# Local attention scores: the order of the small matmuls, and the half of PSUM each head's scores go to

## What is computed

```python
# branch 1: q, k and v averaged over 4 positions, full softmax attention on 144 positions, result repeated 4 times
out_up = np.repeat(sm_attn(q_d, k_d, v_d), 4, axis=2)
# branch 2: full resolution, but only |i - j| < 4
scores = np.where(mask, scale * np.matmul(q, k.transpose(0, 1, 3, 2)), -1e9)
out_local = np.matmul(softmax(scores), v)
x = (out_up + out_local) as (2304 tokens, 512 channels)
y = (silu(x @ w_gate) * (x @ w_val)) @ w_out            # hidden width 1536
out = relu(y @ w2_in) ** 2 @ w2_out                      # hidden width 2048
```

## Time and profile before

| | |
|---|---|
| median of 3 executions | 917.95 us (914.18 to 918.93) |
| the profiled execution's own time | 917.95 us |
| its span, first to last instruction | 916.2 us |
| TensorE (PE) busy | 897.9 us, 98% |
| VectorE / ScalarE / GpSimd busy | 650.9 / 400.5 / 219.4 us |

### The profile page before, as it was taken

The page is one execution under the profiler, slowest core; times in us unless marked ns, Lnnn a source line. Parts: engine busy times, 40 slices in busy tenths (PEclk is TensorE's granted clock), DMA queues, the critical chain, the costliest instruction groups (busy, mean ns, idle before and its releaser), DMA issues.

```text
span 916.2 us, 17274 instructions
## 1 busy us (share of the span) xinstructions
PE 897.9 (98%) x6762; PEld 868.0 (95%) x6762; DVE 650.9 (71%) x1112; ACT 400.5 (44%) x733; POOL 219.4 (24%) x278
## 2 busy tenths in 40 slices
PE   7899999999999999999999999999999999999998
PEld 4589899999999999999999999999999999999998
DVE  7786665653677575887575899585879585878774
ACT  3565454553446252555343545151535241525331
POOL 5884465533352001502000313000403000202000
PEclk9999999999999999999999999999999999999999
DMA  9954333222132020321312220010332020221422
GB/s 233 243 155 118 109 96 108 68 78 95 47 104 70 1 70 24 104 81 35 104 35 92 82 104 1 1 35 2 104 103 70 1 70 1 81 81 40 133 70 70
DMA packets 70881, 71.38 MB, mean 78 GB/s; under 512 B 27280, under 2 KB 58000, under 8 KB 70800
## 3 DMA queue, kind: packets, MB, share of 16 engines
q1 hardware_dynamic: 68496, 65.55, 24.1%
q10 hardware_dynamic: 2304, 4.72, 1.4%
HBM read 56.10 MB, written 14.16 MB: 77 GB/s over the span
## 4 chain that ended last, share of the span: by engine, by line
PE 83%; DVE 6%; ACT 3%; SPq 2%; issue 2%; POOL 2%; DMA 1%; DVEq 0%; ACTq 0%; POOLq 0%
PE mlp_ps L978 13%; PE mlp_ps L980 12%; PE mlp_ps L979 12%; PE sc L978 5%; PE sc L980 5%; PE sc L979 5%; PE xp L978 4%; PE xp L980 4%; PE xp L979 4%; PE sd L978 3%; PE sd L980 3%; PE sd L979 2%; PE tr L978 2%; PE tr L980 2%; PE tr L979 2%
## 5 line engine op out<-in xcount | busy, mean ns | idle before, releaser
L1391 ACT ACTIVATE wh_hi<-hbuf 128x384 fp32r<-128x384 f32 x144 | 70.8, 522 | 79.4 <-DVE hbuf L1677 57.1
L694 POOL TENSOR_TENSOR w_raw<-w_raw 128x256 f32<-128x256 f32 x16 | 13.9, 867 | 355.7 <-DMA w_raw<-w_in 355.7
L1685 DVE TENSOR_TENSOR wh_lo<-hbuf,wh_hi 128x384 fp32r<-128x384 f32 x144 | 76.6, 561 | 24.5 <-ACT wh_hi L1391 21.1
L1640 DVE TENSOR_TENSOR ring<-ring_raw,ring 128x768 fp32r<-128x768 f32 x96 | 91.3, 975 | 0.0
L1340 ACT ACTIVATE ring<-ring_raw 128x768 fp32r<-128x768 f32 x96 | 75.3, 836 | 28.9 <-DVE ring_raw L1634 28.5
L978 PE MATMUL mlp_ps<-ring,w_hi 128*128 128x384 f32 x240 | 80.3, 334 | 0.4 <-ACT snap L1371 0.4
L980 PE MATMUL mlp_ps<-ring,w_lo 128*128 128x384 f32 x240 | 80.2, 334 | 0.0
L979 PE MATMUL mlp_ps<-ring,w_hi 128*128 128x384 f32 x240 | 80.2, 334 | 0.0
L978 PE MATMUL mlp_ps<-wh_hi,w_hi 128*128 128x384 f32 x216 | 73.0, 338 | 2.2 <-DVE ypart L1745 1.2
L979 PE MATMUL mlp_ps<-wh_lo,w_hi 128*128 128x384 f32 x216 | 72.2, 334 | 0.0
L980 PE MATMUL sc<-wh_hi,w_lo 128*128 128x384 f32 x216 | 72.2, 334 | 0.0
(11 more groups left out here) (208 smaller groups left out, 2648.3 us busy)
## 6 DMA issues: line engine op xcount, KB each, us to landing
ring_raw<-x_whole SPq DMA_DIRECT2D x24, 384.0 KB, 3.6
ring_raw<-y_whole SPq DMA_DIRECT2D x24, 384.0 KB, 3.6
qk_sb<-qT SPq DMA_DIRECT2D x16, 288.0 KB, 3.3
qk_sb<-kT SPq DMA_DIRECT2D x16, 288.0 KB, 3.9
v_grp<-v SPq DMA_DIRECT2D x32, 144.0 KB
x_whole<-x_f ACTq DMA_DIRECT2D x16, 288.0 KB, 2.4
y_whole<-ypart SPq DMA_DIRECT2D x3, 1536.0 KB, 6.3
v_win<-v SPq DMA_DIRECT2D x64, 64.0 KB, 2.9
```

The lines of the kernel that those rows point to most:

```text
L694: nc.gpsimd.tensor_tensor(block(5), block(7), block(4), ALU.add).then_inc(s_usum[i], 1)
L1391: nc.scalar.activation(hi[:, f, t, :], hbuf[:, e, :], ACT.Copy).then_inc(s_shhi, 1)
L1640: nc.vector.tensor_tensor(ring[:, SLOTS[g][p], 1, :, :], whole(g, p), ring[:, SLOTS[g][p], 0, :, :].bitcast(F32), ALU.subtract).then_inc(s ...
L1685: nc.vector.tensor_tensor(lo[:, f, t, :], hbuf[:, e, :], hi[:, f, t, :].bitcast(F32), ALU.subtract)\
```

## The change

`local_place` goes away. The scores of head h are now always on partitions 64h onwards, in both banks. The loop over the 20 score matmuls becomes: first all j with head 0 taking t = 0 and head 1 taking t = 1, then all j with head 0 taking t = 1 and head 1 taking t = 0. The values' matmuls keep their order and read their probabilities from the columns that belong to the new place.

```diff
-        def local_place(h, t):
-
-            return h ^ t
-
...
-            for j in range(TJ):
-                for t in range(2):
+            for swap in range(2):
+                for j in range(TJ):
                     for h in range(2):
-                        rows, place = slice(64 * h, 64 * h + 64), 64 * local_place(h, t)
+                        t = h ^ swap
+                        rows = slice(64 * h, 64 * h + 64)
                         s, w = query_at(t, j), window_at(t, j)
-                        last = nc.tensor.matmul(sc[place:place + QT, loc_tile(t, j)],
+                        last = nc.tensor.matmul(sc[64 * h:64 * h + QT, loc_tile(t, j)],
                                                 qk_sb[rows, ring, 0, s:s + QT], qk_sb[rows, ring, 1, w:w + KWIN],
                                                 start=False, stop=(j == TJ - 1))
...
-                        rows, first = slice(64 * t, 64 * t + 64), P * j + 64 * local_place(h, t)
+                        rows = slice(64 * t, 64 * t + 64)
                         last = nc.tensor.matmul(local_bank(i, t)[64 * h:64 * h + 64, QT * j:QT * (j + 1)],
                                                 v_win[rows, ring, j, h, :],
-                                                probsT_l[rows, ring, first:first + QT],
+                                                probsT_l[rows, ring, P * j + 64 * h:P * j + 64 * h + QT],
                                                 start=True, stop=True)
```

## The result

The changed kernel takes 920.96 us in the median (919.59 to 922.07, 11 executions), the kernel before 915.86 us (914.15 to 920.18, 11 executions). The ratio is 1.0053, with a 95% interval from 1.0041 to 1.0065: 4.9 us slower (3.8 to 6.0). The forecast was 924.2 us from 917.95 us, 6.3 us slower. The sign and the mechanism were right, the size was about 1.4 us too large. The measured 920.96 us lies only 0.5 us above the lower end of the forecast range, because the base was taken 2 us too high; the growth itself lies well inside.

What follows compares the result with a forecast made beforehand. TensorE, busy 98% of the span, was taken as the bound after 44 us: 917.95 us plus 6.3 for eleven pairs in the slots, with the opening and the rest at 0, gave 924.2 us; range 920.5 to 929 us.

Steps and rivals of the forecast that it cites:

- Four at once, then two: Local scores: a pair's 40 records go from 10 groups of four to 20 of two, adding 0.57 us a pair.
- The slots: Eleven pairs after 43.9 us, between matmuls that wait for nothing: 11 x 0.57 = 6.3 us added.
- there the addition counts in full: In the slots after 43.9 us, all added score time was to lengthen the kernel: 6.3 us.
- added, but swallowed: Rival, after 44 us: TensorE's waits shrink by 4.6 us, leaving 1.7 us added, 919.7 us; chance 0.08.
- The opening: Pairs 0 to 4, before the slots: 3.4 us of new work hidden by waits, costed at 0.
- The matmul at 43.91 us: At the first slot, waiting for GpSimd's chain without TensorE's part: was to stay there within 0.3 us.
- Two at a time already: Rival, local scores: heads sharing a bank already take turns, so the change costs 0, 918.0 us; chance 0.07.
- Weights no longer ahead: Rival, score groups: weight loads not ahead of the stream, 0.10 us a group, 15.4 us, 933.4 us; chance 0.04.
- The time of before: Whole kernel before the change: 917.95 us, taken as the base of the forecast.

Runs made afterwards that it cites:

- e2: Kernel before with only the changed places (head h always on partitions 64h), loop order as before: ratio 1.0059, 1.12 us for a pair.
- e3: Kernel before with only the changed loop order, places as before: ratio 1.0035, 0.961 us for a pair.
- e4: Kernel before with, inside each j, four quarters still used but neighbours always in different banks: ratio 1.0009, 0.576 us for a pair.
- e7: Kernel before with loop order changed so that ten records in a row go to one quarter of the array: ratio 1.0147.
- e6: Kernel before with the changed places and order for pairs 0 to 4 alone, those of the opening: ratio 0.9997.
- e1: The changed kernel again, unaltered, for a second profile: ratio 1.0041 to the kernel before, median 920.58 us.
- e10: The kernel of e5 once more, against the kernel before: ratio 1.0054.
- e5: Kernel before with the changed places and order for pairs 5 to 15 alone, those of the slots: ratio 1.0068.
- e8: The kernel before again, unaltered, for a second profile: 0.575 us for a pair, 149.74 us from pair 5 to pair 15.
- e11: Kernel before with 8 filler matmuls behind the last values of round 4, ahead of the wait at the first slot: ratio 1.0003.
- e12: Kernel before with 14 filler matmuls behind the last values of round 4, ahead of the wait at the first slot: ratio 1.0010.
- e9: The kernel of e7 once more, for a profile: 930.1 us, 1.73 us for a pair.

## Why the prediction was right, and where not

- **Four at once, then two.** Right, by the starts in both kernels, and by e2, e3, e4 and e7: with the same 640 records, what counts is how many quarters of the array matmuls close to each other in the order use. The interval of a group was taken as 0.057 us and is 0.056; the addition was 0.57 us a pair and is 0.55. A pair of 1.34 us from first start to last end answers to the 1.36 us that were to show it.
- **The slots.** 11 x 0.57 = 6.3 us was forecast; 11 x 0.55 = 6.05 us of stream were added, and 1.0 us came back, 5.06 us net. The term that was mis-sized is "there the addition counts in full". One of the signs named for a wrong forecast, a pair at 1.36 us with a span that doesn't grow by 6 us, has come by the letter: the growth is 4.9 us. The rival *added, but swallowed* holds for a sixth of it: I had set aside the waits for `h_lo` as moving with TensorE, and the 0.35 us one disappeared. The price of that rival, 4.6 us, was too high on its side: of those waits only the 1.0 us for `h_lo` lies in the slots, most of the rest in the passes behind, which keep their length (655.2 and 655.1 us).
- **The opening.** Net 0 was forecast and e6 has 0.9997. The number was right, its main ground was not: the waits for ScalarE of 1.13 to 1.84 us belonged to one execution in which weights landed late, and a second profile of the kernel before would have shown it. GpSimd's chain at the first slot, named but given no price, takes up half of the added work in e1 against e10, and two waits for VectorE, which the prediction counted as well, most of the rest. The matmul at 43.91 us was to stay within 0.3 us. Where TensorE waits for it, it stands between 41.5 and 43.9 us with the scores of before, and between 41.6 and 43.5 us with those of the change, as `v` lands; in the first changed profile, in which TensorE came late, it stands at 47.35 us.
- **Two at a time already.** Refuted: a pair would have stayed at 0.79 us. The reason for it, one bank written from two row halves, costs nothing measurable: e4 against before, and a pair in e2 (1.12 us) against e1 (1.13 us).
- **Weights no longer ahead.** Refuted: 0.10 us stands only between the first two groups, as before.
- **The time of before.** 917.95 us was the median of three; 11 executions have 915.86. Against that base 6.3 us would be 922.2 us.

What remains open is a share of the balance. Executions with a clock of 1.0 average 920.9 us (33 of the changed kernel) and 915.8 us (28 of the kernel before), 5.1 us apart, close to the 5.06 us of the slots. Under 0.999 are 32 of 63 executions before, which average 2.2 us more than those at 1.0, and 4 of 41 after, which average 3.9 us more. That the opening's scores decide how often it happens is shown by the experiments: with the scores of before 8 of 11 (e4) and 7 of 11 (e5 and e10) are under 0.999, with those of the change 1 of 12 (e6) and 1 of 5 (e2), with those of e3, in between, 3 of 12. From these shares I estimate that the change gets back about 0.7 us on average (0.51 x 2.2 less 0.10 x 3.9). By which step is not shown. The clock fell behind the wait at the first slot in e8, e4 and e10, the longer scores shorten that wait, and the fillers ahead of it (e11 and e12, 4 of 23) point the same way; but no experiment changed the wait without giving TensorE other work in the opening.

## What to carry to other kernels

Small matmuls on TensorE stream side by side only if those close to each other in the order differ in the part of the array they use, and both the partitions of the inputs and those of the output choose that part. If one index (here the head) fixes both, half of the array idles: 1.13 us for a pair instead of 0.575. An output place that is the exclusive or of the two indices, as in the kernel before, fills it without an instruction more. In a kernel whose TensorE is busy 98% of the span, a doubling of 0.6 us in each of 11 places came through at five sixths. And waits in the opening have to be read from more than one profile: here the largest total, 4.7 us for ScalarE, was 0.9 us in the next execution of the same kernel.

## What the runs showed of the hardware

- Records for one quarter of the array start before others that stand ahead of them in the loop: in e3 six records early, in e9 30 intervals for 40 records. I had expected starts strictly in order. Whether the engine or the built program changes the order stays open.
- An fp32 matmul of 64 columns on a quarter occupies it for two intervals of 0.056 us, whether one (e9), two (e1) or four quarters (before) are at work. Two that write one bank from different row halves, each to its own half of the partitions, take no longer for it (0.575 us a pair before, 0.576 in e4).
- TensorE's clock fell to the lower of its two levels (1.2 instead of 2.4 GHz) behind the wait of 2.29 us for ScalarE in the first changed profile, for 6.8 us, and behind waits at the first slot of 2.30 us in e8 (for 6.8 us), 2.30 us in e4 and 2.05 us in e10 (for 3.4 us each). From pair 5 to pair 15 that cost 2.0 us in e8, 0.9 in e4 and 1.0 in e10. It did not fall behind waits at the first slot of 0.38 us (before), 0.50 (e1), 0.79 (e3), 0.90 (e2) and 1.80 us (e6), nor behind the 1.84 us for ScalarE in the first profile of the kernel before.
- The first slot starts 5.4 us after GpSimd's first instruction on a landed `v`, in the nine profiles in which GpSimd ends that chain last, and so it stands between 41.49 us (e10) and 43.91 us (the first profile of the kernel before). In the other two, the first changed one and e9, TensorE itself came later.
